# The first expert tile of a fused attention and two-layer expert kernel: its last product in plain 32-bit, its weight splits later, its scores and turns in another place

## The reference, cut to what matters

```python
h = x @ w_in                                  # 2304 x 1024
e = np.exp(h - h_max); sm = e / (e.sum + 1e-9)
solu = h * sm
ln = (solu - mu) / np.sqrt(var + 1e-06) * g_ln
x = ln @ w_out                                # 2304 x 512
out = (sigmoid(x @ w_gate) * (x @ w_val)) @ w_out2
```

## Time and profile before

| | us |
|---|---|
| median of 3 runs | 836.41 |
| lowest and highest | 835.51 and 836.73 |
| the profiled execution's own time | 835.18 |
| its span | 833.4 |
| TensorE busy | 814.7 |
| VectorE busy | 604.4 |
| ScalarE busy | 465.4 |
| GpSimd busy | 20.7 |

### The profile page before, as it was taken

One profiled execution on the slowest core, in us unless ns is written; L12 is line 12 of the kernel. 1 busy time (PEld: TensorE's weight loads), 2 busy tenths in 40 slices (PEclk: granted clock), 3 DMA queues, 4 the chain that ended last, 5 costly groups with the idle time before them and its releaser, 6 DMA issues.

```text
span 833.4 us, 15447 instructions
## 1 busy us (share of the span) xinstructions
PE 814.7 (98%) x5718; PEld 688.1 (83%) x5718; DVE 604.4 (73%) x1460; ACT 465.4 (56%) x965; POOL 20.7 (2%) x35
## 2 busy tenths in 40 slices
PE   7997999999999999999999999999999999999998
PEld 4555777777777778888899999999999999999997
DVE  7988888777777775686656777787677678666654
ACT  7988666666666653463535454564444465444443
POOL 1000000000000000111000000000000000000000
PEclk9999999999999999999999999999999999999999
DMA  7362011111111000100323011122111113111002
GB/s 217 93 194 61 17 52 53 53 52 54 53 50 39 26 17 15 52 1 1 101 77 126 26 51 52 52 61 98 45 52 50 52 42 111 51 52 51 26 1 77
DMA packets 67370, 48.99 MB, mean 59 GB/s; under 512 B 9568, under 2 KB 57952, under 8 KB 67296
## 3 DMA queue, kind: packets, MB, share of 16 engines
q1 hardware_dynamic: 67152, 47.74, 19.2%
q10 hardware_dynamic: 144, 0.26, 0.1%
HBM read 43.27 MB, written 4.72 MB: 58 GB/s over the span
## 4 chain that ended last, share of the span: by engine, by line
PE 89%; DVE 5%; SPq 2%; issue 2%; ACT 1%; DMA 1%; DVEq 0%; ACTq 0%
PE tt_bk L1622 10%; PE tt_bk L1624 10%; PE tt_bk L1623 10%; PE m_bk L1467 9%; PE s_bk L1491 7%; PE o_bk L1491 5%; PE tt_bk L1390 4%; PE s_bk L1674 3%; PE s_bk L1675 3%; PE s_bk L1673 3%; PE o_bk L1398 3%; PE s_bk L1326 3%; PE m_bk L1674 2%; PE m_bk L1675 2%; PE s_bk L1467 2%; PE m_bk L1673 2%
## 5 line engine op out<-in xcount | busy, mean ns | idle before, releaser
L1622 PE MATMUL tt_bk<-xc_hi,wc_hi 128*128 128x384 f32 x476 | 160.0, 336 | 0.0
L1624 PE MATMUL tt_bk<-xc_hi,wc_lo 128*128 128x384 f32 x476 | 160.0, 336 | 0.0
L1623 PE MATMUL tt_bk<-xc_lo,wc_hi 128*128 128x384 f32 x476 | 159.8, 336 | 0.0
L598 ACT ACTIVATE p_nat<-p_nat,negmax 128x512 f32<-128x512 f32 (+2 forms) x144 | 83.0, 578 | 46.6 <-DVE negmax L931 46.6
L1166 DVE TENSOR_TENSOR wc_lo<-wc_raw,wc_hi 128x768 fp32r<-128x768 f32 x72 | 78.3, 1088 | 31.9 <-ACT wc_hi L663 31.9
L1622 PEld LDWEIGHTS tt_bk<-xc_hi,wc_hi 128*128 128x128 f32 x476 | 89.4, 188 | 6.4 <-DVE c_u L1182 0.3
L1623 PEld LDWEIGHTS tt_bk<-xc_lo,wc_hi 128*128 128x128 f32 x476 | 89.4, 188 | 6.1
L1624 PEld LDWEIGHTS tt_bk<-xc_hi,wc_lo 128*128 128x128 f32 x476 | 89.4, 188 | 0.0
L663 ACT CAST wc_hi<-wc_raw 128x768 fp32r<-128x768 f32 x72 | 64.5, 946 | 1.3 <-DVE wc_raw L1160 1.3
L605 ACT COPY pT<-tt_bk 128x512 f32<-128x512 f32 (+1 forms) x87 | 46.0, 554 | 29.2 <-PE tt_bk L1390 27.8
L1390 PE MATMUL tt_bk<-ident,p_nat 128*128 128x128 f32 x400 | 56.0, 277 | 2.6 <-DVE pT L975 1.4
(11 more groups left out here) (219 smaller groups left out, 1773.7 us busy)
## 6 DMA issues: line engine op xcount, KB each, us to landing
wc_raw<-in_moe_w_val SPq DMA_DIRECT2D x36, 256.0 KB, 3.0
wc_raw<-in_moe_w_gate SPq DMA_DIRECT2D x36, 256.0 KB, 3.4
qkT<-in_q SPq DMA_DIRECT2D x15, 288.0 KB, 2.9
v_raw<-in_v SPq DMA_DIRECT2D x16, 256.0 KB, 2.7
qkT<-in_k SPq DMA_DIRECT2D x15, 256.0 KB, 3.2
out<-o_sb SPq DMA_DIRECT2D x15, 256.0 KB, 2.2
w_raw<-in_moe_w_out SPq DMA_DIRECT2D x12, 256.0 KB, 4.7
turned<-in_k SPq DMA_DIRECT2D x32, 72.0 KB, 2.6
```

Of the source, the lines that this page charges most:

```text
L598: nc.scalar.activation(p_tile(g, tile), p_tile(g, tile), ACT.Exp, bias=negmax[:, n:n + 1], scale=-1.0, accum_out=den[:, n:n + 1]).then_inc ...
L1622: mm(o, hi[:, k, c, :], xc_hi[:, j, c, :], start=start and c == 0, stop=False, skip_group_check=True)
L1623: mm(o, hi[:, k, c, :], xc_lo[:, j, c, :], start=False, stop=False, skip_group_check=True)
L1624: last = mm(o, lo[:, k, c, :], xc_hi[:, j, c, :], start=False, stop=c == 1, skip_group_check=True)
```

## The change

The change has four parts.

1. The first tile's last product (`moe_out(0)`, 24 products of split operands) becomes `first_out`: 8 products in plain 32-bit, of the normalised tile times the plain `w_out` from `w2_stage`. The scaling by `g_ln` goes to the tile: VectorE multiplies the transposed tile by it (`first_ln`), in place of ScalarE's two copies `moe_ln(0)` and VectorE's two subtractions.
2. The split `w_out` is then needed one step later, and its splits move. ScalarE's were two in step 4 and six in step 5, VectorE's two in step 4, three in step 5 and three in step 6. Now both engines have two in step 5, three in step 6 and three in step 7.
3. In step 5 TensorE makes the third scores behind twelve products of the tile, not six, and the last scores and turns 2 to 6 behind all 24; turns 0 and 1 stand behind eighteen. Copy 4 of pair 4 goes from VectorE to ScalarE.
4. In step 6 TensorE makes all 24 products of the tile before turn 0, and the pieces of `first_out` stand between the turns.

```diff
-        W2_HI_MID, W2_HI_X, W2_HI_TILE, W2_HI_END = {4: (0, 1)}, {5: (2, 3, 4)}, {5: (5, 6)}, {5: (7,)}
-        W2_LO_PHI, W2_LO_TILE = {4: (0, 1)}, {5: (2, 3, 4), 6: (5, 6, 7)}
+        W2_HI_X, W2_HI_TILE, W2_HI_END = {6: (2, 3, 4), 7: (5, 6, 7)}, {5: (0,)}, {5: (1,)}
+        W2_LO_MAX, W2_LO_ROWS, W2_LO_VAR = {6: (2,), 7: (5, 6)}, {5: (0,), 6: (3,), 7: (7,)}, {5: (1,), 6: (4,)}
...
+            def first_ln():
+                dve.wait_ge(g_in, 16)
+                for n in range(2):
+                    dve.wait_ge(lnt_ready, n + 1)
+                    c = slice(512 * n, 512 * n + 512)
+                    nc.vector.tensor_tensor(u_even[:, c].rearrange("p (f k) -> p f k", f=4),
+                                            t_bk[n][:, :].rearrange("p (f k) -> p f k", f=4),
+                                            g_col[:, 4 * n:4 * n + 4].unsqueeze(2).broadcast_to([P, 4, P]),
+                                            ALU.mult).then_inc(ln_lo_ok, 1)
...
                 moe_rows(t)
                 moe_stats(t)
                 if t == 0:
                     unit_max(g + 1, 0)
                     unit_max(g + 1, 1)
+                for f in W2_LO_VAR.get(g, ()):
+                    split_w2(f)
                 moe_var(t)
...
+            def first_out(f0, f1):
+                if f0 == 0:
+                    pe.wait_ge(ln_lo_ok, 2)
+                    pe.wait_ge(w2_in, 16 * FB)
+                for f in range(f0, f1):
+                    last = mm(y_bank(False), u_even[:, f * P:(f + 1) * P], w2_stage(f)[:, 0, :], start=f == 0,
+                              stop=f == FB - 1)
...
+                if t == 1:
+                    moe_hidden(t, 12, 24)
+                    turn_p(g - 1, 0)
+                    turn_p(g - 1, 1)
+                    pe.wait_ge(max_ok, NU * g + NU - 1)
+                    first_out(0, 2)
+                    turn_p(g - 1, 2)
+                    turn_p(g - 1, 3)
+                    first_out(2, 4)
+                    turn_p(g - 1, 4)
+                    turn_p(g - 1, 5)
+                    first_out(4, 6)
+                    turn_p(g - 1, 6)
+                    first_out(6, 8)
```

More of the change, by code:

```diff
@@ L73, in act_fills @@
             return list(range(NF))
-        return [0, 2, 5, 6] if g == HP else [0, 2, 4, 5, 6]
+        return [0, 2, 4, 5, 6]
     def dve_fills(g):
@@ L774, in early_step @@
                     exp_tile(g, n)
-                for f in W2_HI_MID.get(g, ()):
-                    split_w2(f)
                 exp_tile(g, 6)
@@ L791, in step @@
                 keep_both(g - 2)
-                if t == 1:
-                    moe_ln(t - 1)
                 if t in OWN:
@@ L801, in step @@
                 if g < PAIRS:
-                    for n in range(2, 8):
+                    for n in range(2, 6):
+                        exp_tile(g, n)
+                    if t == 0:
+                        keep_pt(g - 1, 0)
+                    for n in range(6, 8):
                         exp_tile(g, n)
@@ L805, in step @@
                     feature_relu(g + 1)
-                keep_pt(g - 1, 0)
+                if t:
+                    keep_pt(g - 1, 0)
                 if t == 0:
@@ L809, in step @@
                 keep_pt(g - 1, 2)
+                if t == 0:
+                    keep_pt(g - 1, 4)
                 if t == 1:
@@ L814, in step @@
                 moe_exp(t)
-                if 4 in act_fills(g - 1):
+                if t:
                     keep_pt(g - 1, 4)
@@ L1062, in early_step @@
                     split_w1(c)
-                for f in W2_LO_PHI.get(g, ()):
-                    split_w2(f)
             def step(g, t):
@@ L1072, in step @@
                 normalize(g - 1, 1)
-                if t:
+                if t == 1:
+                    first_ln()
+                elif t:
                     moe_ln_low(t - 1)
@@ L1093, in step @@
                 if t == 0:
-                    split_w2(W2_LO_TILE[g][0])
                     unit_max(g, 6)
-                    split_w2(W2_LO_TILE[g][1])
                 keep_pt(g - 1, 1)
-                if t < 2:
-                    split_w2(W2_LO_TILE[g][2 if t == 0 else 0])
+                if t == 0:
+                    keep_pt(g - 1, 3)
+                for f in W2_LO_MAX.get(g, ()):
+                    split_w2(f)
                 moe_max(t)
-                keep_pt(g - 1, 3)
-                if t == 0:
-                    keep_pt(g - 1, 4)
-                if t == 1:
-                    split_w2(W2_LO_TILE[g][1])
-                    split_w2(W2_LO_TILE[g][2])
+                if t:
+                    keep_pt(g - 1, 3)
+                for f in W2_LO_ROWS.get(g, ()):
+                    split_w2(f)
                 moe_rows(t)
@@ L1492, in moe_out @@
                 if m1 == 3 * FB:
+                    last.then_inc(y_ready, 1)
+            def first_out(f0, f1):
[5 more added lines that the diff above has]
+                              stop=f == FB - 1)
+                if f1 == FB:
                     last.then_inc(y_ready, 1)
@@ L1555, in step @@
                     hidden_begins(g, t)
+                    moe_hidden(t, 6, 12)
                 if t in OWN and g < PAIRS:
@@ L1559, in step @@
                     hidden_begins(g, t)
-                if t != 1:
                     moe_hidden(t, 6, 12)
@@ L1563, in step @@
                     scores(g, 2)
+                if t != 1:
+                    moe_hidden(t, 12, 18)
+                    turn_p(g - 1, 0)
+                    turn_p(g - 1, 1)
+                    moe_hidden(t, 18, 24)
                 if t == 0:
                     scores(g, 3)
-                m = (15, 21) if t == 0 else (18, 24)
-                moe_hidden(t, 12, m[0])
-                turn_p(g - 1, 0)
-                turn_p(g - 1, 1)
-                moe_hidden(t, m[0], m[1])
-                turn_p(g - 1, 2)
-                turn_p(g - 1, 3)
-                if t == 0:
-                    moe_hidden(t, 21, 24)
-                if t:
+                if t != 1:
+                    turn_p(g - 1, 2)
+                    turn_p(g - 1, 3)
+                if t > 1:
                     if g < PAIRS:
@@ L1580, in step @@
                     moe_out(t - 1, 0, 6)
-                turn_p(g - 1, 4)
-                turn_p(g - 1, 5)
-                if t:
+                if t != 1:
+                    turn_p(g - 1, 4)
+                    turn_p(g - 1, 5)
+                if t > 1:
                     moe_out(t - 1, 6, 12)
-                turn_p(g - 1, 6)
-                if t:
+                if t != 1:
+                    turn_p(g - 1, 6)
+                if t > 1:
                     moe_out(t - 1, 12, 24)
+                if t == 1:
+                    moe_hidden(t, 12, 24)
+                    turn_p(g - 1, 0)
+                    turn_p(g - 1, 1)
+                    pe.wait_ge(max_ok, NU * g + NU - 1)
+                    first_out(0, 2)
+                    turn_p(g - 1, 2)
+                    turn_p(g - 1, 3)
+                    first_out(2, 4)
+                    turn_p(g - 1, 4)
+                    turn_p(g - 1, 5)
+                    first_out(4, 6)
+                    turn_p(g - 1, 6)
+                    first_out(6, 8)
                 if t and g < PAIRS:
```

2 lines of the change are left out of this document (1 added, 1 removed).

## The result

The changed kernel takes 837.69 us (median of 22 runs, 835.96 to 839.73), the one before 836.14 us (22 runs beside them, 835.01 to 838.5). The ratio is 1.0019, 95% interval 1.0013 to 1.0025: 1.1 to 2.1 us slower, and inside what the prediction called the same. The forecast was 837.8.

What follows compares the result with a forecast made beforehand. TensorE, busy 814.7 of 833.4 us, was taken as the bound. Gains of 2.7 and 0.5 to 0.7, losses of 1.7, 2.0, 0.3 and 1.56 were given as 1.4 us longer: 836.6 profiled, median 837.8; 8-in-10 range 835.3 to 839.2.

Steps and rivals of the forecast that it cites:

- Start and order of step 5: Step 5: first product 1.2 us earlier, and with the new order pair 6's first scores 2.7 us earlier, at 77.7.
- the row sums took the gain back: End of step 5: row sums only 1.0 us earlier, TensorE idles about 1.6 us, so the gain shrinks to 1.0.
- The weight block before the variance: End of step 5: block 1's low part delays VectorE's variance by 1.65 us; TensorE idles 2.0 us before the transposes.
- The rival in which this wait is hidden: Step 5's variance: ScalarE reaches block 1 early, transposes start at 85.0; 835.5 us, chance 0.14.
- The plain product: Step 6: eight plain products at 0.885 us take 7.1 us where 24 split ones took 5.5; 1.56 us more.
- The two bounds, 3.5 and 8.7: Step 6: eight plain products take 3.5 us at 0.44 each from below, 8.7 us by the first scores from above.
- the rival of the cheap product: Step 6: plain products cost 0.44 us each, the lower bound; 834.3 us, chance 0.07.
- the rule of four passes: Step 6: a true 32-bit product takes four passes; eight are 32 against 24, 7.4 us, sum 838.1.
- The sum as listed: Steps 5 and 6: the prediction's listed gains and losses, stated to come to 1.4 us longer.
- VectorE's list as the bound: Step 6, the slower rival: VectorE's lateness goes straight to the end; 838.6 to 839.2 us, chance 0.24.
- Step 7: Three more splits on each engine there, 2.1 us on VectorE, fit into its waits and cost nothing.

Runs made afterwards that it cites:

- e3_order5: The changed kernel with TensorE's order and the copies of step 5 as before the change; 838.84 us (6 runs), ratio 1.0036 to the kernel before.
- e6_var_order5: The edits of e1_var and e3_order5 together, on the changed kernel; 835.9 us (11 runs), ratio 0.9996 to the kernel before.
- e1_var: The changed kernel with VectorE's low part of weight block 1 moved from before step 5's variance to step 6's maximum; 835.55 us, ratio 0.9989 to before.
- e1_again: The kernel of e1_var profiled once more with no edit; 835.67 us in one execution.
- e2_plain: The kernel before with only the plain product added (`first_ln` and `first_out`), weight splits and orders as before; 837.67 us, ratio 1.0018 to before.
- e4_order6: The changed kernel with step 6's old order, turns 0 to 3 between the tile's products, `first_out` behind them; 839.69 us (5 runs), ratio 1.0041 to before.
- after_again: The changed kernel profiled once more with no edit; 839.85 us in one execution.

## Why the prediction came true, step by step

The measured times are those of the trace of after less 1.30.

| step | predicted | measured |
|---|---|---|
| first product of the first tile | 65.6 | 65.83 |
| last scores of step 5 | 72.8 | 73.09 |
| turn 3, and the wait before it | 75.1, 1.1 | 75.36, 0.97 |
| turn 4 | 76.0 | 76.26 |
| first scores of pair 6 | 77.7 | 78.11 |
| row sums | 79.0 | 79.26 |
| wait before the weighting | 1.6 | 1.53 |
| scaling of block 1 | 83.4 | 83.69 |
| variance | 84.85 | 85.10 |
| first tile's transposes, and the wait | 87.0, 2.0 | 87.25, 1.87 |
| second tile's products | 87.9 | 88.10 |
| turns 0 and 1 | 95.0 | 95.07 |
| `first_out` | 96.0 | 96.25 |
| last scores of step 6 | 105.3 | 105.29 |

**Start and order of step 5.** Right in kind; the gain was put 0.2 to 0.4 too high: the first product came 1.0 us earlier, not 1.2, and the first scores 2.3, not 2.7. One reading was more than its row says: for the 1.36 us before the first product the row names no releaser ("issue"), and that VectorE's low part ended it is inferred from its end at 66.72, 0.1 us before. Of the gain that is missing, the wait for the transfer of `v_raw` (0.2) is one part; turns 5 and 6, which I let go at the pace of the copies, hold a wait of 0.33 more. That had no effect, for the row sums took the gain back as predicted; in the traces of e3_order5 and e6_var_order5 this order is worth 0.14 us or less by the end of step 6.

**The weight block before the variance.** This is the step on which the forecast turned, and e1_var with e1_again shows it: 2.2 us of step 6 go when that one low part goes, and with the 0.2 for `v_raw` taken off the transposes come 2.0 us earlier, as forecast. The rival in which this wait is hidden named 835.5; e1_var, where it is in fact gone, took 835.55.

**The plain product.** Eight take 1.82 + 1.72 + 1.72 + 1.81 = 7.07 us (from each start to the next row; 97.55 to 99.37 is the first), against 7.1. The two bounds, 3.5 and 8.7, are both off, and with them the rival of the cheap product. What I undervalued is the form that goes: the 24 split products took not 5.5 but 5.9 in the trace of before (96.89 to 98.36, 99.22 to 100.69 and 100.94 to 103.89), since the first behind each turn costs 0.1 more, which I had counted in step 5 and not here. The difference is 1.2; the turns take 0.14 more where plain products stand between them. From the turns to the last scores it is 9.04 against 7.72: the term was 1.32, not 1.56 (e2_plain: 1.25). By the rule of four passes, which the prediction takes from the Trainium skill (page FP8 and Floating Point Precision, section TensorE Precision Notes), the eight would take 7.4, an estimate; the trace has 4 x 0.23 = 0.92 for none of them, but 0.86 to 0.91, so the rule is near and the row of the weighting products nearer.

**Two small errors cancel.** The norm came 0.25 late and the plain product was 0.25 cheaper: hence 105.29 against 105.3. That the agreement is so close is luck; single steps were off by up to 0.4 us.

**The sum as listed.** The list of gains and losses in the prediction does not add up to its 1.4. Its terms (2.7 gained, 1.7 and 2.0 lost, 0.5 to 0.7 gained, 0.3 and 1.56 lost) give 2.2 to 2.4. The 1.4 comes from the timeline alone, in which the stretch from the second tile's products to `first_out` is 8.1 us where before it was 9.28 to turn 2: 1.2 us gained, the new wait counted in. The traces have 8.15, so the timeline was right and the list wrong.

**VectorE's list as the bound.** It did not come: turn 0 of step 6 waited for nothing, and `first_out` 0.26 us against the 0.3 predicted. VectorE's scaling of the memory part was done by 96.1, TensorE came to turn 0 at 96.37: the margin was 0.2, as the prediction had it. It was near, and the 0.3 us before `first_out` are its beginning. With the old order of step 6 this bound would be reached, as the estimate under e4_order6 says.

**Step 7.** No new wait, as predicted.

**From the trace to the median.** Steps 5 and 6 give +1.40, the median +1.55. The sum has no term for a fall of the granted clock behind the new waits, which cost 1.1 us in after_again. The profiled execution was 1.0 above the forecast of 836.6 for it, which is the start's 1.30 less 0.3 behind step 6: I had taken the start of before's profile, and the clock of that stretch is chance. A slow stretch as in after_again may have its part in the median. Four of the 22 runs had a mean clock of 0.992 (839.1 us on average), none of the 60 runs of the kernel before that stand beside the experiments was under 0.993; but these runs have no trace, so that is inferred and not shown.

## What to carry to other kernels

Ask of every instruction that is put into an engine's list what stands directly behind it and when its own operand is ready: one instruction of 0.7 us, ahead of a variance that did not need it, cost 2.2 us, while in the traces a larger reordering of the matrix engine in the same step was worth 0.14. Follow a gain to the next point where another engine hands over (here the row sums) before booking it. When executions differ by chance at the start, compare the length of the steps concerned, not the whole.
